# Attention, routed experts and gated convolution on one core: transposed inputs and whole-array scores replaced by host layouts, one pair of score banks and two banks of transposed probabilities

## The reference

```python
rel = pos[:, None] - pos[None, :]
mask_plain = (rel >= 0) & (rel < window)                                   # window = 32
mask_dil = (rel >= 0) & (rel < window * dilation) & (rel % dilation == 0)  # dilation = 4
scores = np.where(masks[None], scale * np.matmul(q, k.transpose(0, 1, 3, 2)), -1000000000.0)
attn = np.exp(scores - np.max(scores, axis=-1, keepdims=True))
attn = attn / (np.sum(attn, axis=-1, keepdims=True) + 1e-09)
x = np.matmul(attn, v)                        # 2304 tokens of 512 columns, all heads side by side
...
# routing: per token an expert; a token whose local gate is 0.5 or more keeps the one before
e = fresh_e if s == 0 or local_gate[b, s] < 0.5 else prev_e
out[b, s] = p[e] * (np.maximum(x[b, s] @ w1[e], 0.0) @ w2[e])              # 8 experts, 512 x 1024
...
gate = sigmoid(causal 5-tap convolution of x over s)
result = (gate * (x @ w_val)) @ w_out
```

## Time and profile before

| | us |
|---|---|
| median of 3 runs (660.03 to 663.44) | 661.99 |
| span of the profiled execution, which is its own time here | 663.2 |
| PE busy | 585.3 (88%) |
| DVE, POOL, ACT busy | 300.0, 290.3, 226.4 |
| attention, up to the last logits | about 180 |
| routing, up to `token_idx` | about 33 |
| experts | about 300 |
| convolution and projections | about 150 |

### The profile page before, as it was taken

One profiled execution on the slowest core, in us unless ns is written; L12 is line 12 of the kernel. 1 busy time (PEld: TensorE's weight loads), 2 busy tenths in 40 slices (PEclk: granted clock), 3 DMA queues, 4 the chain that ended last, 5 costly groups with the idle time before them and its releaser, 6 DMA issues.

```text
span 663.2 us, 12185 instructions
## 1 busy us (share of the span) xinstructions
PE 585.3 (88%) x3425; PEld 499.4 (75%) x3426; DVE 300.0 (45%) x888; ACT 226.4 (34%) x498; POOL 290.3 (44%) x209
## 2 busy tenths in 40 slices
PE   3896999989808699999999999999998487999988
PEld 2785979778706588887888888888886377898966
DVE  3583788848487111121121121121121559988510
ACT  2573565736000112122122122122122377674421
POOL 8150414200470664586235656375864625522210
PEclk9796999969557989999999999999998669899989
DMA  5858577491992699899597788779876421211112
GB/s 117 136 140 178 124 155 163 126 243 46 280 313 87 200 388 323 300 306 366 209 303 243 262 273 256 252 248 387 290 263 210 143 73 47 70 67 48 49 47 79
DMA packets 99357, 129.53 MB, mean 195 GB/s; under 512 B 46848, under 2 KB 57504, under 8 KB 99328
## 3 DMA queue, kind: packets, MB, share of 16 engines
q1 hardware_dynamic: 72240, 63.98, 32.8%
q0 software_dynamic: 19824, 52.98, 25.5%
q10 hardware_dynamic: 7264, 12.21, 5.4%
HBM read 105.80 MB, written 23.33 MB: 195 GB/s over the span
## 4 chain that ended last, share of the span: by engine, by line
PE 50%; SPq 16%; DMA 12%; DVE 8%; issue 7%; POOL 5%; ACT 2%; POOLq 0%; DVEq 0%; ACTq 0%
PE bank L1178 39%; SPq L356 11%; DMA w_high<-in_moe_w 4%; POOL w_low L565 3%; SPq L352 2%; PE bank L1383 2%; DMA x_sorted<-gathered 2%; DVE gate_acc L981 2%; PE bank L1251 2%; PE bank L1215 1%; POOL gathered L626 1%; DMA gathered<-x_tokens,token_idx 1%; DMA x_tokens<-x_dil 1%; PE bank L1261 1%; PE bank L1436 1%
## 5 line engine op out<-in xcount | busy, mean ns | idle before, releaser
L565 POOL TENSOR_TENSOR w_low<-stage,w_high 128x2048 f32 (+1 forms) x32 | 146.9, 4604 | 68.4 <-DMA stage<-in_moe_w 38.1
L1028 ACT ACTIVATE probs<-shifted,negmax 96x128 f32<-96x128 f32 x192 | 61.3, 390 | 58.0 <-DVE negmax L774 58.0
L1178 PE MATMUL bank<-w_high,h_high 128*128 x184 | 74.7, 406 | 3.7 <-DVE h_low L940 2.3
L1178 PE MATMUL bank<-w_high,x_high 128*128 x184 | 75.3, 409 | 2.7 <-DVE x_low L931 1.7
L1178 PE MATMUL bank<-w_high,x_low 128*128 x184 | 73.0, 397 | 0.0
L1178 PE MATMUL bank<-w_high,h_low 128*128 x184 | 72.8, 395 | 0.0
L1178 PE MATMUL bank<-w_low,x_high 128*128 x184 | 72.7, 395 | 0.0
L1178 PE MATMUL bank<-w_low,h_high 128*128 x184 | 72.3, 393 | 0.0
L1066 ACT CAST x_high<-bank 128x512 fp32r<-128x512 f32 x25 | 14.7, 587 | 156.1 <-PE bank L1348 148.9
L931 DVE TENSOR_TENSOR x_low<-bank,x_high 128x512 fp32r<-128x512 f32 x25 | 17.3, 691 | 111.3 <-ACT x_high L1066 104.1
L1080 ACT CAST h_high<-bank 128x1024 fp32r<-128x1024 f32 x25 | 25.4, 1015 | 120.1 <-PE bank L1383 120.1
(11 more groups left out here) (174 smaller groups left out, 1256.4 us busy)
## 6 DMA issues: line engine op xcount, KB each, us to landing
stage<-in_moe_w SPq DMA_DIRECT2D x32, 1024.0 KB, 7.5
w_high<-in_moe_w POOLq DMA_DIRECT2D x16, 2048.0 KB, 10.3
y_sorted<-y_sb ACTq DMA_DIRECT2D x25, 256.0 KB
x_sorted<-gathered SPq DMA_DIRECT2D x21, 256.0 KB, 13.3
x_in<-x_sorted ACTq DMA_DIRECT2D x21, 256.0 KB, 6.3
out<-o_sb SPq DMA_DIRECT2D x18, 256.0 KB
vwin<-in_v POOLq DMA_DIRECT2D x28, 128.0 KB, 3.3
q_rows<-in_q SPq DMA_DIRECT2D x16, 144.0 KB, 4.1
```

The source lines that it names most:

```text
L565: g.tensor_tensor(low, stage[:, c % 2, :], high.bitcast(F32), ALU.subtract).then_inc(split_done, 1)
L1028: a.activation(probs[:, j % 2, u, :], shifted[:, j % 2, u, :], ACT.Exp, bias=negmax[:, j % 2, u:u + 1], scale=-1.0).then_inc(exp_done, 1)
L1178: ins = mm(dst, l, r, start=first and i == 0, stop=last and i == 2)
```

## The change

The host now hands over q and k already transposed (two heads on 128 rows), v already cut into windows with a column of ones, and the gate and convolution weights by partition. So the kernel has no `transpose_qk`, no copies of k and q, no memsets of `vwin` and `k_pair`; a pair's q and k are one DMA each and a batch's v is one. The inputs lie double buffered by batch.

`scores` is now four matmuls of 128 columns that are 64 rows deep, one for each head and block. Head 0 of the pair writes bank 0, head 1 bank 1, in every step: there is one pair of score banks, and `scores` of step j waits until DVE has read all of step j-1 (before: j-2). The transposed probabilities keep two banks (2 and 3), used for nothing else.

The x work is spread: each step transposes its own 2 x 96 rows of x (`transpose_out`, banks 6 and 7), ACT copies them, and `gate_logits` makes 2 matmuls of 9 columns. DVE takes the logits (`take_logits`), adding the two pairs of a kind. Of the dilated half only the 9 logit columns travel through DRAM and back, no longer 256 columns of x. The steps are written out, 48 of them, with no hardware loop.

On POOL the loads of expert 0 and its four splits now start when 30 of the 48 steps are normalised, and the constants for the routing come after them, behind waits for the last logits and for the last store of the plain half of x. The diff, cut to what matters here:

```diff
@@ SP
+            def load_pair(b, n, q_too=True):
+                if b >= 2:
+                    sp.wait_ge(scores_done, STEPS * (b - 2) + PAIR_STEPS * (n + 1))
+                if q_too:
+                    sp.dma_start(qT[:, b % 2, n, :], q_t[b, n]).then_inc(qk_loaded[b % 2][n], 16)
+                sp.dma_start(kT[:, b % 2, n, :], k_t[b, n]).then_inc(qk_loaded[b % 2][n], 16)
...
+            def store_dil(b):
...
+                sp.wait_ge(lg_taken, STEPS * b + STEPS // 2)
...
+                sp.wait_ge(lg_stored, 16 * len(QUERY_PIECES) * (b + 1))
+                if b > 0:
+                    sp.wait_ge(logits_ready, b)
+                sp.dma_start(lg_back[:, :, :], lgs.rearrange("o (t p) c -> p (o t) c", p=QB)).then_inc(lg_loaded, 16)
+
+            def store_plain(b):
+                sp.wait_ge(normed, STEPS * (b + 1))
...
+            load_pair(0, 0, q_too=False)
+            load_pair(0, 1)
+            load_v(0)
...
@@ POOL
-            load_rows(po, k_rows, k, 0, 0, which=(1,), loaded=first_loaded)
-            g.memset(vwin[:, :, :, :, HD:OUTC], 1.0)
-            g.memset(vwin[0:WINDOW, :, 0, :, 0:HD], 0.0)
-            g.memset(vwin[0:WINDOW, :, NQ // 2, HEADS // 2:, 0:HD], 0.0)
...
+            po.wait_ge(normed, 2 * STEPS + STEPS // 2)
+            load_high(0, 0, 0)
+            load_high(0, 0, 1)
+            for c in range(CHUNKS):
+                split(0, c, 0)
+            po.wait_ge(logits_ready, BATCH)
+            po.wait_ge(plain_stored, 16 * BATCH)
...
-            po.wait_ge(back_loaded, 16 * BATCH)
-            load_high(0, 0, 0)
-            load_high(0, 0, 1)
-            for c in range(CHUNKS):
-                split(0, c, 0)
@@ DVE
+            def take_logits(m):
...
+                    d.tensor_copy(part, got).then_inc(lg_taken, 1)
+                else:
+                    dve.wait_ge(lg_taken, m - PAIR_STEPS + 1)
+                    d.tensor_tensor(part, got, part, ALU.add).then_inc(lg_taken, 1)
...
+            for s in range(ALL_STEPS + 5):
+                if s >= 5:
+                    take_logits(s - 5)
+                if s < ALL_STEPS:
+                    mask_and_max(s)
+                if 2 <= s < ALL_STEPS + 2:
+                    norm(s - 2)
@@ ACT
+            for s in range(ALL_STEPS + 4):
+                if s >= 4:
+                    copy_x(s - 4)
+                if s < ALL_STEPS:
+                    exps(s, (0, 1))
+                if 1 <= s <= ALL_STEPS:
+                    copy_probs(s - 1)
+                if s < ALL_STEPS:
+                    exps(s, (2, 3))
@@ PE
+            def scores(j):
+                b, n, i = place_of(j)
                 if i == 0:
...
+                    pe.wait_ge(qk_loaded[b % 2][n], 32 * (b // 2 + 1))
+                if j >= 1:
+                    pe.wait_ge(shifted_done, UNITS * j)
                 for w in range(PW):
                     t = PW * i + w
-                    ins = mm(bank[0:QB, j % 2, w * 2 * KB:(w + 1) * 2 * KB], qT[:, n % 2, t * QB:(t + 1) * QB],
-                             k_pair[:, n % 2, :, t * QB:t * QB + KB], start=True, stop=True)
+                    for hh in range(2):
+                        rows = slice(hh * HD, (hh + 1) * HD)
+                        ins = mm(bank[0:QB, hh, w * KB:(w + 1) * KB],
+                                 qT[rows, b % 2, n, t * QB:(t + 1) * QB],
+                                 kT[rows, b % 2, n, t * QB:t * QB + KB], start=True, stop=True)
...
+            def transpose_out(j):
...
+                pe.wait_ge(normed, j + 1)
...
+            def gate_logits(j):
...
+                pe.wait_ge(x_copied, j + 1)
...
+            for s in range(ALL_STEPS + 5):
+                if s < ALL_STEPS:
+                    scores(s)
+                if 1 <= s <= ALL_STEPS:
+                    transpose_probs(s - 1)
+                if 2 <= s <= ALL_STEPS + 1:
+                    times_v(s - 2)
+                if 3 <= s <= ALL_STEPS + 2:
+                    transpose_out(s - 3)
+                if s >= 4 and s < ALL_STEPS + 4:
+                    gate_logits(s - 4)
```

More of the change, by code:

```diff
@@ L249, in build @@
         small_loaded = sem("small_loaded")
[L250 to L256, removed]
+        qk_loaded = [[sem(f"qk_loaded{i}_{n}") for n in range(PAIRS)] for i in range(2)]
+        v_loaded = [sem(f"v_loaded{i}") for i in range(2)]
         scores_done = sem("scores_done")
@@ new lines, in _ @@
+            sp.dma_start(convw[:, :, :], conv_t.rearrange("p (k t) -> p k t", k=KD)).then_inc(small_loaded, 16)
+            load_pair(0, 2)
+            load_pair(0, 3)
+            for n in range(PAIRS):
+                load_pair(1, n)
+            load_v(1)
+            for b in range(BATCH):
+                store_dil(b)
+                if b == 2:
+                    load_raw(sp, 0, 0)
+                    load_raw(sp, 0, 1)
+                store_plain(b)
+                if b + 2 < BATCH:
+                    for n in range(PAIRS):
+                        load_pair(b + 2, n)
+                    load_v(b + 2)
+                if b == 2:
@@ new lines, in norm @@
+                if b > 0 and i == 0 and n == 2:
+                    dve.wait_ge(plain_stored, 16 * b)
+                dve.wait_ge(den_ready, 2 * m + 2)
+                h = PAIR_HEAD[n]
+                dst = (x_plain if h < 4 else x_dil)[:, PW * i:PW * (i + 1), (h % 4) * HD:(h % 4 + 2) * HD]
+                d.tensor_tensor(dst.rearrange("p t (h c) -> p h t c", c=HD),
+                                o[:, :, 0:HD].rearrange("p (h t) c -> p h t c", h=2),
+                                rden[:].rearrange("p (h t) -> p h t", h=2).unsqueeze(3)
+                                .broadcast_to([QB, 2, PW, HD]), ALU.mult).then_inc(normed, 1)
@@ L1043, in _, with exps @@
-            load_rows(act, k_rows, k, 0, 0, which=(0,))
-            for j in range(-2, LOOP[0]):
-                step(0, j)
-            with act.Fori(0, BATCH - 1) as b:
-                for j in LOOP:
-                    step(b, j)
-            for j in LAST:
-                step(0, j)
+            def exps(j, units):
+                if units[0] == 0 and j >= 2:
+                    act.wait_ge(probs_transposed, j - 1)
+                for u in units:
+                    act.wait_ge(shifted_done, UNITS * j + u + 1)
+                    a.activation(probs[:, j % 2, u, :], shifted[:, j % 2, u, :], ACT.Exp,
+                                 bias=negmax[:, j % 2, u:u + 1], scale=-1.0).then_inc(exp_done, 1)
@@ new lines, in gate_logits @@
+            def gate_logits(j):
+                b, n, i = place_of(j)
+                if j == 0:
+                    pe.wait_ge(small_loaded, 32)
+                pe.wait_ge(x_copied, j + 1)
+                for w in range(PW):
+                    at = PW * QB + w * LOGC
+                    ins = mm(bank[0:QB, 6 + j % 2, at:at + LOGC], xT_sb[:, j % 2, w * QB:(w + 1) * QB],
+                             wg[:, PAIR_HEAD[n] // 2, :], start=True, stop=True)
+                ins.then_inc(x_multiplied, 1)
```

402 lines of the change are left out of this document (116 added, 286 removed).

## The result

The changed kernel takes 674.94 us (673.06 to 677.37, four runs), the kernel before 661.03 beside it (660.03 to 663.44, four runs): a ratio of 1.021, 95% interval 1.016 to 1.025. It is slower, by 1.6 to 2.5%, where 603 us was predicted. The profiled execution has a span of 671.5.

What follows compares the result with a forecast made beforehand. PE was taken to bound attention and experts. An earlier `top` (-47.6) and shorter routing (-11.5) gave -59.1 on the profiled 663.2: 604.1; that execution lying 1.2 above the median, 602.9, written 603 us, range 588 to 620.

Steps and rivals of the forecast that it cites:

- Three steps of it bring step 3 to 15.1, and with one at 2.36 step 4 is at 17.5: Attention's start: three loops of about 3.2 us at the lower clock, then steps of 2.36 us, step 47's scores at 119.0.
- experts and after: Stage behind the routing, bounded by PE: code and PE work unchanged, with 2 us either way from the clock at entry.
- The clock stays low: Rival, 3%: 64-row scores with short waits keep PE at 1.2 GHz in the attention, 4.7 us a step, 707 us total.
- overlap: Rival, 27%: two heads' scores run side by side on PE, steps of 2.13 to 2.25 us, 592 to 598 us total.
- The step on PE: One attention step's PE work: scores, transposes, `times_v`, `transpose_out` and `gate_logits` sum to 2.34 us, 2.36 with joints.
- The loop through the one pair of banks: Attention: scores wait for the previous step's masks, a loop of 2.3 us, just below PE's 2.36, costing nothing.
- The drain: Rival, 13%: changes between 64-row and full matmuls cost PE 0.3 us a step in the attention, 617 us total.
- The start: Before the attention: first scores decided by the first pair's data at 5.5 us, instead of 11.65; late `v` charged nothing.
- The end of the attention: From step 47's scores at 119.0 through norm and POOL's constants to `top` at 133.1 instead of 180.70: -47.6 us.
- The routing: DVE's routing: three operations shrink from 4.43, 4.09 and 3.99 us to about 0.35 each, -11.5 us.
- rden: Rival, 8%: this or another DVE operation in the attention is blocked by POOL's splits, +4 to +16 us, up to 619.

Runs made afterwards that it cites:

- k5: Changed kernel with both heads' scores matmuls reading rows 0 to 63, so head 1's scores are those of head 0; 713.61 us, one run.
- e4: Kernel before with scores as four matmuls of 64 rows and 128 columns and one pair of score banks; 715.47 us, one run.
- k7: Kernel before with scores as four matmuls of 128 rows and 128 columns and one pair of score banks; 660.81 us against 662.65, one run.
- e2: Changed kernel with 24 dense matmuls on a constant tile on PE ahead of the first scores; 604.59 us, one run.
- k9: Changed kernel with eight dense matmuls once, ahead of the transposes of step 24; 636.34 us, four runs, ratio 0.965 to the kernel before.
- e1: Changed kernel with scores matmuls reading all 128 rows instead of 64, each summing both heads; 605.08 us, one run.
- k6: Changed kernel with 8 dense matmuls ahead of the first scores, POOL's constants late; 596.88 us, one execution.
- k8: Changed kernel with 16 dense matmuls ahead of the first scores and POOL's constants made early; 596.29 us, six runs, ratio 0.898 to the kernel before.
- k12: Changed kernel with POOL's constants early and eight dense matmuls ahead of the transposes of step 3; 593.6 us, six runs, ratio 0.904 to the kernel before.
- e3: Changed kernel with one dense matmul in each step, ahead of the transposes of the probabilities; 603.22 us, one run.
- k10: Changed kernel with 8 dense matmuls ahead of the first scores and POOL's constants early; 671.84 us, six runs, ratio 1.022 to the kernel before.
- k13: Same kernel as k6, 8 dense matmuls ahead of the first scores, run again; 670.57 to 678.18 us in six executions, ratio 1.023 to the kernel before.

## Why the prediction was wrong, by its own steps

**The step that failed is the clock.** "Three steps of it bring step 3 to 15.1, and with one at 2.36 step 4 is at 17.5": the low steps of the start were to be followed by 44 at 2.36. They never were. Step 47's scores stand at 187.46 instead of 119.0, which is 68.5 us; 42 x (3.98 - 2.36) = 68.0 of it are the steps from 5 to 47. With 1.7 more from there to `top`, it is 70.2 late. The rest of the sum: routing -12.0 instead of -11.5, experts and after 447.4 instead of 449.7. 604.1 + 70.2 - 0.5 - 2.3 = 671.5, the span.

**The rival had it, at 3%.** "The clock stays low" gave 707 us with a step of 4.7; the step is 3.98 because the rival "overlap" is true as well (1.10 for the scores, where k5 without overlap has 1.95). With the step as measured the rival's own sum gives 603 + 44 x (3.98 - 2.36) = 674. No row before had the price of overlapping scores at that clock. What spoke against the rival was the clock of 1.00 from 24.8 to 48 "with steps of nearly the same list". Two faults lie in that. The list was not nearly the same: its scores were 128 rows deep, and e4 against k7 shows that this alone is 55 us in the kernel before. And the row shows that a list keeps a clock that it has, which is true of the changed list too (e2, k9), and says nothing on whether it comes to it. The kernel before had rows that ask this question: from 168.6 to 180.4 us its trace shows PE busy at a clock of 0.50 throughout, with matmuls of 9 columns and transposes, and 135 to 145 has PE busy for 10.00 of 10 us at 0.55.

```profile
168.60:180.40 11.80, 11.71 (x72) 11.35 (x72) 3.36 (x7) 0.00 (x0) 4.97 (x3) 0.50 1.02 325
```

Both stand behind a wait of PE (1.06 us before 168.63, 3.29 before 134.59). But PE was then busy for 11.71 of 11.80 us at 0.50, and from 135 to 144 without a gap at 0.50 as well, and I read both as passing.

**The step on PE was right** at the clock that it was made for: 2.36 predicted, 2.37 in e1, where scores don't overlap; 2.18 with overlap, inside the rival's 2.13 to 2.25 (its floor of 0.65 us for the scores is not one: they issue in 0.61). Its time, 592 to 598, is what k6, k8 and k12 have (596.9, 596.3, 593.6), with their dense matmuls and, in the last two, early constants.

**The loop through the one pair of banks** costs nothing, as predicted: in e2 PE waits nowhere over 0.1 us behind the first steps, even at 2.18, and k7 measures it in the kernel before. The one longer wait through the banks in these traces is k8's of 0.81 us, and its cause is the way of the dilated logits through DRAM, which the prediction called hidden.

**The drain**, the rival in which a change between 64-row and full matmuls costs PE time, was priced at 0.3 us a step, two changes of 0.15 (0.80 - 0.65 in the earlier trace rows), and gives the 617 us that the range was drawn from. No run shows that term. At the half clock, behind eight records of the same columns, 2.02 us busy in both, the transposes start after 1.95 us in k5 (64 rows, 101.94 to 103.89) and after 1.81 in e1 (128 rows, 8.21 to 10.02): 0.14 apart, and a change is not the only difference. At the full clock no run separates it: the four transposes issue in 0.38 us behind 64-row scores (60.67 to 61.05 in e2) and in 0.34 behind 128-row ones (14.96 to 15.30 in e1), and what a change takes inside the 0.61 us of the overlapping scores isn't known. The step of 2.18 holds it, whatever it is.

**The start**: 5.16 us, predicted 5.5. `v` was not late. **The end of the attention**: from step 47's scores to `top` 15.8 us, 14.1 predicted, with the constants last, as said. At the higher clock e1 has 13.7 and e2 16.0, so the 1.7 isn't shown to be the clock's. The pieces that the prediction names up to the end of the norm add to 7.05 us, not to 6.5. **The routing**: the three operations have 0.26, 0.34 and 0.31 us, 0.35 predicted each. **`rden`** was not blocked; it takes 0.17 beside the splits. But the premise that DVE beside the splits reads at most one operand from SBUF missed `logits<-lg_plain,lg_back`, which reads two. It fell between the splits here (0.21 us). In k5 it started at 194.02 beside one and took 3.24.

**What stays open.** Why the changed list doesn't raise the clock is not shown beyond this: the depth of the scores decides it (e1 against k5, e4 against k7), not overlap, waits or the pair of banks, and one dense matmul a step makes up for it (e3). Each of these is one execution, and k6 shows that one can differ from six of the same kernel. Two pairs that agree and four executions of the changed kernel at the lower clock speak against luck. Why k6's one execution kept the clock and twelve of k10 and k13 lost it is open too. Their three traces have the same waits of 1.16 and 0.55 us in the first steps; they differ in whether the clock was up before these or came up during them. The waits alone don't take it: k8's trace has the same two (at 11.18 and 12.90), with the clock up before them, and keeps it. That the waits lose it is supported by k9 and k12, where none follow, and not shown: a kernel that removes the waits and leaves the eight at the start wasn't tried. What stands ahead of the eight differs as well: nothing on PE until 4.3 us in k13, 12 us of steps in k12. That rival is untested.

## What to carry to other kernels

Before pricing PE's work from one stretch, ask which level of the clock the durations there belong to, and whether the new list would raise the clock itself: this list kept the full clock for 109 us (e2) and didn't reach it in 167 us of busy PE. Compare a known operation's mean before and after (here `times_v`, 255 to 359 ns), since a printed 1.00 stood over half-clock durations here (20 to 187 us). If a list of half-depth matmuls stays low, a few us of dense matmuls on a constant tile, put where PE has no more waits ahead, bought 12% here (674.9 to 593.6 in k12, its early constants included); at the very start the same ones mostly failed. That it is the place past the waits that counts is not shown.

## What the runs showed that I had not expected

- PE busy for all of 167 us (20 to 187) at the half clock, and the same instructions at the full clock for 102 us once some 3 us of dense matmuls had raised it (k12; in k9 the step goes from 3.98 to 2.18 us).
- Matmuls in rows 0 to 63 and 64 to 127 with different banks run side by side: eight records in 1.10 us against 1.95 in k5 at the half clock, and 0.61 against 0.92 at full depth (e1, 14.04 to 14.96) at the full clock.
- After the same wait for `x_back`, of some 6 us, the list with 128-row scores had the full clock back within 4 us (k7), and the one with 64-row scores not again in the attention (e4).
- DVE operations of 4 us in the earlier trace rows take 0.3 us when POOL's TENSOR_TENSORs run at another time.
